# Moving and splitting the weight chunks' low parts in a routed expert stage

## The reference

```python
logits = x @ w_gate
expert_idx = np.argmax(logits, axis=1)
probs = softmax(logits);  gate_w = probs[rows, expert_idx]
for e in range(8):
    mask = expert_idx == e
    h = np.maximum(x[mask] @ w1[e], 0.0)          # 512 -> 1024
    out[mask] = gate_w[mask, None] * (h @ w2[e])   # 1024 -> 512
```

## Time and profile before

| what | us |
|---|---|
| median of 3 runs | 1511.38 (1510.37 to 1511.91) |
| profiled execution | 1509.39 |
| its span, first to last instruction | 1507.7 |
| TensorE busy | 1473.6, 98% of the span |
| VectorE, ScalarE, GpSimd busy | 979.4, 713.0, 630.7 |
| expert loop, turns 3 to 38 | from 1058.6 to about 1479 |

### The profile page before, as it was taken

One profiled execution on the slowest core, in us unless ns is written; L12 is line 12 of the kernel. 1 busy time (PEld: TensorE's weight loads), 2 busy tenths in 40 slices (PEclk: granted clock), 3 DMA queues, 4 the chain that ended last, 5 costly groups with the idle time before them and its releaser, 6 DMA issues.

```text
span 1507.7 us, 28846 instructions
## 1 busy us (share of the span) xinstructions
PE 1473.6 (98%) x8070; PEld 1274.8 (85%) x8071; DVE 979.4 (65%) x1877; ACT 713.0 (47%) x1512; POOL 630.7 (42%) x681
## 2 busy tenths in 40 slices
PE   7999999999999999999999999999999899999997
PEld 6999999999978888888888888887888778888885
DVE  5688888888825374655637465535677777777663
ACT  5688788788812122121212212143566566656442
POOL 6676676676810021020202102021667776665221
PEclk9999999999999999999999999999999999999999
DMA  7354344344430202021120202134424433321110
GB/s 254 115 142 107 104 107 107 103 108 127 109 122 0 71 15 84 0 84 28 56 70 14 84 0 84 29 131 153 167 96 141 163 116 130 125 73 49 40 48 23
DMA packets 84601, 134.67 MB, mean 89 GB/s; under 512 B 50016, under 2 KB 50272, under 8 KB 80338
## 3 DMA queue, kind: packets, MB, share of 16 engines
q1 hardware_dynamic: 76978, 114.01, 25.2%
q0 software_dynamic: 7584, 20.17, 4.2%
HBM read 104.26 MB, written 30.94 MB: 90 GB/s over the span
## 4 chain that ended last, share of the span: by engine, by line
PE 67%; DVE 1%; DMA 1%; POOL 1%; issue 1%; ACT 1%; POOLq 0%; ACTq 0%; DVEq 0%
PE bank L166 65%; PE bank L1669 1%; POOL big L1104 1%; DVE xs L1466 1%; DMA arena<-rows_scratch,ids 1%; ACT arena L1244 0%; DMA out<-arena,ids 0%; DVE arena L1451 0%; PE bank L1600 0%; PE bank L1705 0%; PE bank L1619 0%; PE bank L1608 0%; ACT big L809 0%; PE bank L1594 0%; DVE xs L1428 0%
## 5 line engine op out<-in xcount | busy, mean ns | idle before, releaser
L166 PE MATMUL bank<-big,xs 128*128 (+1 forms) x2088 | 492.6, 395 | 14.7 <-DVE big L609 8.1
L166 PEld LDWEIGHTS bank<-big,xs 128*128 128x128 f32 x2088 | 391.7, 189 | 96.7 <-issue 15.8
L166 PE MATMUL bank<-xs,big 128*128 128x512 f32 x1728 | 397.4, 391 | 2.7 <-PEq L215 2.7
L166 PEld LDWEIGHTS bank<-xs,big 128*128 128x128 f32 x1728 | 324.7, 188 | 70.3 <-issue 2.9
L166 PE MATMUL bank<-big 128*128 128x512 f32 (+1 forms) x1632 | 325.8, 348 | 2.0 <-POOL big L305 1.4
L166 PEld LDWEIGHTS bank<-big 128*128 128x128 f32 (+1 forms) x1632 | 255.8, 165 | 36.2 <-POOL big L305 1.7
L1021 POOL TENSOR_TENSOR arena<-arena 128x512 f32<-128x512 f32 x32 | 39.8, 1255 | 440.5 <-DMA arena<-rec_scratch 440.2
L1397 DVE TENSOR_TENSOR arena<-arena,bank 128x512 f32<-128x512 f32 x72 | 49.4, 686 | 246.0 <-PE bank L166 246.0
L1157 ACT COPY arena<-bank 128x512 f32<-128x512 f32 x72 | 42.3, 587 | 306.9 <-PE bank L166 302.6
L1322 DVE CUSTOM_DVE_ANT_0 arena<-arena 128x512 f32<-128x512 f32 x256 | 159.5, 688 | 14.9 <-ACT arena L1177 14.7
L1451 DVE TENSOR_SCALAR arena<-bank,gate 32x256 f32<-32x256 f32 x288 | 138.9, 482 | 44.5 <-PE bank L166 40.1
(11 more groups left out here) (175 smaller groups left out, 1395.0 us busy)
## 6 DMA issues: line engine op xcount, KB each, us to landing
arena<-we SPq DMA_DIRECT2D x32, 1024.0 KB, 4.8
kqraw<-kq SPq DMA_DIRECT2D x32, 576.0 KB, 3.8
rows_scratch<-arena SPq DMA_DIRECT2D x36, 256.5 KB
xT_scratch<-arena SPq DMA_DIRECT2D x32, 288.0 KB
arena<-v SPq DMA_DIRECT2D x64, 128.0 KB, 2.4
arena<-xT_scratch SPq DMA_DIRECT2D x8, 1024.0 KB, 5.4
arena<-rec_scratch SPq DMA_DIRECT2D x64, 128.0 KB, 3.8
arena<-w3T SPq DMA_DIRECT2D x8, 512.0 KB, 3.4
```

Of the source, the lines that this page charges most:

```text
L166: ins = nc.tensor.matmul(out, left[a], right[b], start=first and n == 0, stop=last and n == 2)
```

## The change

1. A chunk's low part is made in two halves of 1024 columns: GpSimd makes the upper half (`w_lo`), VectorE the lower one (new semaphore `w_lo2`). TensorE and SyncE wait for both.
2. On ScalarE the chunks stand at the end of a tile's turn, behind `turned_h_high`, where they stood between `rows_high` and `next_gate`. VectorE's halves stand at the end of its turn, behind `turned_h_low`.
3. GpSimd's turn g is now: scatter of tile g-2, the chunks of turn g-1, gather of tile g+2.
4. The table `CH` is computed by other rules. For the same tile counts it gives, for turns 3 to 28: 1 1 1 1 1 1 1 1 1 1 2 2 1 1 1 1 0 1 1 1 1 0 1 1 1 1, and none after it: 26 chunks again.

```diff
@@ SyncE
                     sp.wait_ge(w_lo, SLOTS * i + u - SLOTS + 1)
+                    sp.wait_ge(w_lo2, SLOTS * i + u - SLOTS + 1)
                     load(SLOTS * i + u, u)
@@ GpSimd
-            def weights(c):
+            def weights(c, n=HW):
...
-                pool.tensor_tensor(ring[:, 1, ds(at, CW)], ahead[:, ds(slot, CW)],
-                                   ring[:, 0, ds(at, CW)].bitcast(F32), ALU.subtract).then_inc(w_lo, 1)
+                pool.tensor_tensor(ring[:, 1, ds(at, n)], ahead[:, ds(slot, n)],
+                                   ring[:, 0, ds(at, n)].bitcast(F32), ALU.subtract).then_inc(w_lo, 1)
...
-            weights(CPE + 1)
-            scatter(1)
+            weights(CPE + 1, CW)
 
             def period(g):
+                scatter(g - 2)
+                tile_chunks(pool, g - 1, weights)
                 gather(g + 2)
-                tile_chunks(pool, g, weights)
-                scatter(g - 1)
@@ ScalarE
             def tile(g):
                 relu_moved(g)
                 rows_high(g + 1, False)
-                tile_chunks(act, g, weights)
                 next_gate(g + 1)
                 turned_h_high(g)
+                tile_chunks(act, g, weights)
@@ VectorE
                 turned_h_low(g)
+                tile_chunks(dve, g, weights)
+
+            def weights(c):
+                at, slot = dve.snap((c % RING) * CW), dve.snap((c % SLOTS) * CW)
+                dve.wait_ge(w_hi, c + 1)
+                dve.tensor_tensor(ring[:, 1, ds(at, HW)], ahead[:, ds(slot, HW)],
+                                  ring[:, 0, ds(at, HW)].bitcast(F32), ALU.subtract).then_inc(w_lo2, 1)
@@ the table (one of its rules)
-            linked(dve.tensor_scalar(ch, ch, 1.0 / CPE, 1.0, ALU.mult, ALU.min), base)
+            linked(dve.tensor_scalar(ch, ch, 1.0 / CPE, 1.0 / CPE, ALU.mult, ALU.add), base)
+            linked(dve.scalar_tensor_tensor(ch, ch, 1.0, ex, ALU.min, ALU.add), base)
@@ TensorE
                         pe.wait_ge(w_lo, CPE * e + c * FF // CW + 1)
+                        pe.wait_ge(w_lo2, CPE * e + c * FF // CW + 1)
```

More of the change, by code:

```diff
@@ L854, in stage2 @@
         w_hi, w_lo = m["w_hi"], m["w_lo"]
+        w_lo2 = sem("s3_w_lo2")
+        HW = CW // 2
         lg_mm, lg_shift, lg_exp = sem("s2_lg_mm"), sem("s2_lg_shift"), sem("s2_lg_exp")
@@ L1085, in _ @@
             for g in range(1, FIRST):
-                pool.wait_ge(gate_set, g)
+                pool.wait_ge(gate_set if g == 1 else gate_saved, g)
                 pool.wait_ge(xtr_mm, g)
@@ L1098, in _ @@
             pool.wait_ge(rows_out, 16 * BQ * NB)
-            def weights(c):
-                at, slot = ((c % RING) * CW, (c % SLOTS) * CW) if isinstance(c, int) else (
-                    pool.snap((c % RING) * CW), pool.snap((c % SLOTS) * CW))
+            def weights(c, n=HW):
+                at, slot = ((c % RING) * CW + CW - n, (c % SLOTS) * CW + CW - n) if isinstance(c, int) else (
+                    pool.snap((c % RING) * CW + CW - n), pool.snap((c % SLOTS) * CW + CW - n))
                 pool.wait_ge(w_hi, c + 1)
-                pool.tensor_tensor(ring[:, 1, ds(at, CW)], ahead[:, ds(slot, CW)],
-                                   ring[:, 0, ds(at, CW)].bitcast(F32), ALU.subtract).then_inc(w_lo, 1)
+                pool.tensor_tensor(ring[:, 1, ds(at, n)], ahead[:, ds(slot, n)],
+                                   ring[:, 0, ds(at, n)].bitcast(F32), ALU.subtract).then_inc(w_lo, 1)
             gather(FIRST)
@@ L1111, in _ @@
             pool.wait_ge(tabs, 2)
-            weights(CPE)
+            weights(CPE, CW)
             gather(FIRST + 1)
-            weights(CPE + 1)
-            scatter(1)
+            weights(CPE + 1, CW)
             def period(g):
+                scatter(g - 2)
+                tile_chunks(pool, g - 1, weights)
                 gather(g + 2)
-                tile_chunks(pool, g, weights)
-                scatter(g - 1)
             last = tiles(pool, period, 2)
-            last1, last2 = last_of(pool, 1), last_of(pool, 2)
+            last1, last2, last3 = (last_of(pool, k) for k in (1, 2, 3))
+            scatter(last3)
+            tile_chunks(pool, last2, weights)
             keep_gate(last)
+            scatter(last2)
             tile_chunks(pool, last1, weights)
-            scatter(last2)
-            tile_chunks(pool, last, weights)
             scatter(last1)
@@ L1230, in h_high @@
                     act.wait_ge(w_lo, NCH)
+                    act.wait_ge(w_lo2, NCH)
                 elif g > 0:
@@ L1282, in _ @@
             relu(last)
-            tile_chunks(act, last, weights)
             h_high(last)
@@ L1473, in tile @@
                 turned_h_low(g)
+                tile_chunks(dve, g, weights)
[4 more added lines that the diff above has]
+                                  ring[:, 0, ds(at, HW)].bitcast(F32), ALU.subtract).then_inc(w_lo2, 1)
             dve.sem_inc(h_turned, 1)
+            dve.sem_inc(w_lo2, CPE + 2)
             turns(dve, turn)
@@ L1539, in _ @@
             early_w2 = W1C / CPE
-            linked(dve.tensor_scalar(ch, ch, 1.0 / CPE, 1.0, ALU.mult, ALU.min), base)
[L1542 to L1552, removed]
+            one, two = slice(1, last_g + 1), slice(2, last_g + 2)
+            most = slice(0, last_g)
+            linked(dve.tensor_scalar(ch, ch, 1.0 / CPE, 1.0 / CPE, ALU.mult, ALU.add), base)
@@ new lines, in _ @@
+            linked(dve.scalar_tensor_tensor(ch, ch, 1.0, ex, ALU.min, ALU.add), base)
+            linked(dve.tensor_scalar_add(ch, ch, 1.0), base)
+            linked(dve.scalar_tensor_tensor(ahead_of[:, most], ex[:, one], early_w2, ex[:, two], ALU.add, ALU.max), base)
+            linked(dve.scalar_tensor_tensor(ch[:, most], ahead_of[:, most], early_w2, ch[:, most], ALU.add, ALU.max), base)
+            linked(dve.scalar_tensor_tensor(ahead_of[:, most], ex[:, most], early_w2, ex[:, one], ALU.add, ALU.min), base)
@@ L1553, in _ @@
+            linked(dve.scalar_tensor_tensor(ch[:, most], ahead_of[:, most], 2.0, ch[:, most], ALU.add, ALU.min), base)
+            linked(dve.scalar_tensor_tensor(ch[:, 1:last_g], ahead_of[:, 0:last_g - 1], 2.0 + 2.0 / CPE,
                                             ch[:, 1:last_g], ALU.add, ALU.min), base)
-            linked(dve.scalar_tensor_tensor(ch[:, 2:last_g], ahead_of[:, 1:last_g - 1], 2.0 + 2.0 / CPE,
-                                            ch[:, 2:last_g], ALU.add, ALU.min), base)
@@ L1557, in _ @@
-            linked(dve.scalar_tensor_tensor(ch[:, 0:last_g], ex[:, 1:last_g + 1], early_w2,
-                                            ch[:, 0:last_g], ALU.add, ALU.max), base)
+            linked(dve.tensor_scalar_min(ch[:, FIRST:FIRST + 1], ch[:, FIRST:FIRST + 1], (CPE + FIRST) / CPE), base)
+            linked(dve.scalar_tensor_tensor(ahead_of[:, most], ex[:, most], early_w2, ex[:, one], ALU.add, ALU.max), base)
+            linked(dve.scalar_tensor_tensor(ch[:, most], ahead_of[:, most], early_w2, ch[:, most], ALU.add, ALU.max), base)
@@ L1559, in _ @@
             linked(dve.tensor_scalar(ch, ch, float(CPE), float(NCH), ALU.mult, ALU.min), base)
             linked(dve.tensor_scalar_min(tabf[:, 0], tabf[:, 0], float(E - 1)), base)
-            linked(dve.memset(tabf[:, 2, FIRST - 1:FIRST], float(CPE + FIRST - 1)), base)
+            linked(dve.memset(tabf[:, 2, FIRST - 2:FIRST], float(CPE + FIRST - 1)), base)
             linked(dve.tensor_copy(tabf[:, 3], ends[:, E - 1:E].to_broadcast([P, GMAX])), base)
@@ L1567, in _ @@
             linked(dve.tensor_scalar_add(tabf[:, 3, 3:4], tabf[:, 3, 0:1], -3.0), base)
+            linked(dve.tensor_scalar_add(tabf[:, 3, 4:5], tabf[:, 3, 0:1], -4.0), base)
             dve.tensor_copy(m["tab"][:, 0:ROW], m["tabf"][:, 0:ROW]).then_inc(tabs, 1)
@@ L1692, in second_product @@
                         pe.wait_ge(w_lo, CPE * e + W1C + j * DM // CW + 1)
+                        pe.wait_ge(w_lo2, CPE * e + W1C + j * DM // CW + 1)
                     if j % DC == 0:
```

## The result

The changed kernel takes 1528.93 us (median of 4 runs, 1527.65 to 1529.76) against 1510.88 us for the kernel before in the same comparison: ratio 1.0118, with an interval of 1.010 to 1.0136. It is 1.2% slower. The forecast was 1514.9 us with a range of 1506 to 1528. The direction was right, the size was not: +18 us came where +3.5 us were forecast, and the time lies just above the range.

The account below looks back on a forecast made before the run. TensorE, busy for 98% of the span, was taken to bound the kernel. Winning 11.3 us and adding 14.8 us of new waits gave +3.5 us: 1512.9 us for the profiled execution, 1514.9 us for the median, range 1506 to 1528.

Parts of the forecast that it names:

- The gain: Expert stage: TensorE's waits of 3.86 and 1.96 us and the clock's fall go, all 11.3 us lost are won.
- The ring: Waits through ScalarE and VectorE once a turn: 11.99 us with one copy, against TensorE's 11.36; new waits 14.8 us in all.
- The step that failed: ScalarE's table reads and waits in front of the copy at the turn's end: taken as hidden beside L1251, costing nothing.
- The upper bound: If the table reads are not hidden, 0.43 us each turn: ring 12.42 us, in all 25 us of new waits.
- the forecast's own sum: TensorE's new waits over the loop's chunk turns, less slack and what turns without a chunk give back: 14.8 us.
- reads that show: Rival: ScalarE's table reads show in each turn, ring 12.4 us, 25 us lost, 1525 us; chance 0.17.
- TensorE's second wait per chunk: TensorE's wait for work that ends a turn before its use, except behind double turns, where the ring is late: nothing.
- the rival in which GpSimd comes first: VectorE's half ends later behind GpSimd's: ring 12.8 us, 34 us lost, 1534 us; chance 0.06.
- the 5.0 us forecast: New waits in the two turns with two chunks, where the ring takes 2.49 us more than TensorE does.
- The rival of the clock: TensorE's clock falls behind the double turns after waits of 2.5 us; two falls give 1520 us; chance 0.08.
- The forecast for VectorE's half: Subtraction of 1.23 us at VectorE's turn's end: hidden beside ScalarE's relu, with 1.6 us to spare.

Follow-up runs that it names:

- experiment 2: Kernel before with only the split: GpSimd makes 1024 columns of a chunk's low part, VectorE the others at its turn's end; 1498.84 us, ratio 0.9935.
- experiment 3: Changed kernel with ScalarE's two table reads moved ahead of next_gate, where it is idle; 1508.13 us, ratio 0.9999 to the kernel before.
- experiment 4: Changed kernel with two more, unused table reads on ScalarE between turned_h_high and the copy; 1562.74 us, ratio 1.0354 to the kernel before.
- experiment 5: Changed kernel with ScalarE's copy in the loop only 1024 columns wide, leaving out part of the computation; 1507.77 us, ratio 0.999 to the kernel before.
- experiment 7: Changed kernel with ScalarE's copy back between rows_high and next_gate and the table of before; 1508.28 us, ratio 0.9984 to the kernel before.
- experiment 6: Changed kernel without VectorE's half, GpSimd making a chunk's whole low part; 1531.16 us, ratio 1.0135 to the kernel before.
- experiment 1: Kernel before with one line changed: the gather of tile 2 waits for gate_saved instead of gate_set; 1507.88 us, ratio 0.9992.

## Why the prediction was right in its direction and wrong in its size

**The gain.** Taking the 3.86 us, the 1.96 us and the fall of the clock away was forecast, and it happened: no turn's L1469 is longer than 1.23 us. That the moves were needed for it, which the prediction left open, is not so: experiment 2 gets 10.4 of the 11.3 us with the split alone.

**The ring.** Right. ScalarE's copy at the turn's end closes a ring that bounds every one-chunk turn. Experiments 3, 4, 5 and 7 change one of its lengths, or take the copy out, and the turn follows each time.

**The step that failed: "what reads the table and waits in front of a copy ... I take it as hidden".** The term was mis-sized: taken as 0, bounded by 0.43, measured 0.67 us per turn. The 0.43 us of the earlier trace rows was read as "1.02 us from L1200's start", and compared with L1251's 1.05. Both lengths are true, but 1.02 is not how long the reads take. The trace does show the reads by themselves, against what the prediction says: they are operations of ScalarE's sequencer (ACTq), line 823. Here they are in the turn of the earlier trace rows before, and in the turn with one chunk after (count, shortest, median and longest in ns, start of the first and of the last):

```profile
L823 ACTq FUSED_REGOPS  x4: 51/104/152, 1303.4 to 1304.4; - x4
L823 ACTq TENSOR_LOAD <-tab x2: 277/278/279, 1303.5 to 1304.1; - x2
```

```profile
L823 ACTq FUSED_REGOPS  x4: 51/104/152, 1157.6 to 1158.6; - x4
L823 ACTq TENSOR_LOAD <-tab x2: 277/282/286, 1157.7 to 1158.3; - x2
L823 ACTq SEQ_ASSERT  x2: 18/18/18, 1158.2 to 1158.8; - x2
```

From the first of them to the copy L809 are 1.7 us in both kernels (1303.4 to 1305.11, and 1157.6 to 1159.28). About 1.2 us are the two reads, 0.5 us the branches and addresses behind them. Before, the sequencer began 0.7 us ahead of L1200 (1304.09), while the engine was still busy with its relu pieces. After, it has to wait for VectorE's transposition first and begins together with L1255, so 1.72 - 1.05 = 0.67 us show. The upper bound was therefore no bound, and the trace of the kernel before had the length that was missing. The Trainium skill (DMA: Bandwidth & Descriptors, Latency and other measured facts) has a `tensor_load` at not less than about 600 ns. The estimate by that floor, 1.2 us for two, was near in its sum, but the load by itself takes 0.28 us here, and the 0.5 us behind the reads were not in the estimate; the measurement decides.

In numbers, here is the forecast's own sum with 12.62 for the ring: the surplus over TensorE's turn is 1.26 instead of 0.63 us, so 10 x 1.26 - 1.6 = 11.0, then 4 x 1.26 = 5.0 and twice 4 x 1.26 - 1.2 = 3.8. With the double turns as measured, 4.94 + 1.80 = 6.7, that is 30.4 us against 32.4 lost. Most of the rest is again the reads, since a turn without a chunk reads the table too: its ring is 10.97 us (L1255 at 1275.40 and 1286.37, with 0.82 us of "issue" in front of L1248) and not 10.1, so it gives back 0.39 us and not 1.2, twice. The sum was built right and was fed a wrong length. The chance for "reads that show", 0.17, was given to the case that came true.

**The double turns.** "TensorE's second wait per chunk ... nothing" was wrong. I had let GpSimd's halves take 2.31 us, and had put the two engines' exclusion only into the rival in which GpSimd comes first. VectorE came first, as argued, and GpSimd then waited: 3.40 us for a half, 6.70 for two. TensorE's waits of 2.86 and 1.51 us for it, and the fall of the clock (24 matmuls in 7.31 instead of 5.73 us), are not what the two turns lost, though: ScalarE's ring took 14.73 us in each, and 2 x (14.73 - 11.36) = 6.7 us is all of it. Of the 14.73 us, 12.62 are the ring with one copy, 1.81 the second copy, and 0.3 come from the exclusion: VectorE's second half ended at 1204.01, its three relu pieces at 1205.50, and L1431 could not follow L1203 at 1205.2. So 0.63 us of reads and 0.3 us of exclusion per turn stand between the 5.0 us forecast and the 6.7. The rival of the clock came true in one of two turns, and cost nothing in this kernel, since TensorE was not what set the pace.

**The forecast for VectorE's half** (hidden, with 1.6 us to spare) held in turns with one chunk: it ends at 1162.81, three pieces later VectorE waits 1.25 us for ScalarE, and experiment 6 shows the same turn without it.

**A part of the change was missed**, the first gathers' line. In the profiles it is worth 2.4 us, in the runs of experiment 1 about 0.6 us, which is not clear of nothing. Without it the forecast would have been a little further off.

## What to carry to other kernels

An engine that is idle for much of the time can still have no room for an instruction at a given place: add up the ring of waits from one turn's instruction to the same one in the next turn, and put new work where the engine waits for another one, not behind that wait. Count as part of the ring what the engine's sequencer does between two instructions (reads of a table, branches); how much of it shows depends on how long before it the sequencer was free, so a gap measured in one place is no bound for another place. Look for the sequencer's own operations in the trace, and take their length. Read such a table early, where the engine waits anyway: here that alone gave back the change's whole loss (the split alone is another 0.6% faster). And before you put a price on a wait of TensorE or on a fall of its clock, see which engine sets the pace: where a ring does, TensorE can make up for both.

## What the runs showed of the hardware

- Two reads of a table on ScalarE's sequencer, with the branches and addresses behind them, take 1.7 us, before and after the change. The load in a read is 0.28 us, the whole read about 0.6 us; each further read of the same kind costs 0.53 us (2.77 against 1.72 us for four and two).
- The sequencer runs ahead of its engine: before the change it began the reads 0.7 us ahead of the start of the instruction in front of them. Behind a wait it cannot, and after the change it began them together with that instruction.
- A subtraction on GpSimd and one on VectorE with both inputs in the core's memory exclude each other in both directions: GpSimd's half is 2.39 us alone and 3.40 us beside VectorE's of 1.23 us, and VectorE's is 2.77 us behind GpSimd's. Two pairs that start together take 6.7 us.
- How long TensorE waited does not tell by itself whether its clock falls. It fell after waits of 2.86 us (after the change) and 2.12 us (experiment 7), not after 1.51 us in the first and 2.53 us in the second. In experiment 4 it fell after seven of the fourteen waits of 1.81 to 1.87 us (24 matmuls in 7.3 us) and not after the other seven (5.7 us).
